# GpSimd takes over sums of weights and products of gated tiles, and the due times around them move

## The reference

```python
out_d = sm_attn(q_d, k_d, v_d)                    # means over 4 positions
attn = softmax(where(|i - j| < 4, scale * q @ k.T, -1e9))
x = (repeat(out_d, 4) + attn @ v)                 # 2304 x 512
x = ((x @ w1) * (x @ w2)) @ w3 @ w_out            # d_ff 1024
h = maximum(maximum(x @ u1, x @ u2), x @ u3)      # d_ff 768
out = h @ u_out
```

## Time and profile before

| | us |
|---|---|
| median of 3 runs | 718.35 (716.84 to 719.42) |
| the profiled execution | 716.85, span 715.1 |
| PE busy | 681.6 (95%) |
| DVE busy | 464.2 (65%) |
| POOL busy | 316.2 (44%) |
| ACT busy | 274.8 (38%) |
| DMA, share of 16 engines | 74.2% |

### The profile page before, as it was taken

The page is one execution under the profiler, slowest core; times in us unless marked ns, Lnnn a source line. Parts: engine busy times, 40 slices in busy tenths (PEclk is TensorE's granted clock), DMA queues, the critical chain, the costliest instruction groups (busy, mean ns, idle before and its releaser), DMA issues.

```text
span 715.1 us, 16905 instructions
## 1 busy us (share of the span) xinstructions
PE 681.6 (95%) x6848; PEld 648.1 (91%) x6848; DVE 464.2 (65%) x843; ACT 274.8 (38%) x590; POOL 316.2 (44%) x280
## 2 busy tenths in 40 slices
PE   8999989799968999989999999999999999999998
PEld 7878878798868999889999999999999999999997
DVE  4465788878877674466545575457775677756673
ACT  5455334434433444356444355123241222412221
POOL 6989354654755422254022235024382243812441
PEclk9999999989999999999999999999999999999999
DMA  9884577778764877997999857996769766697632
GB/s 311 265 276 135 141 211 219 208 211 225 225 170 142 265 229 255 327 313 246 306 349 353 276 205 275 414 399 231 229 231 399 246 220 229 245 406 245 214 142 88
DMA packets 97820, 180.04 MB, mean 252 GB/s; under 512 B 7760, under 2 KB 47952, under 8 KB 96976
## 3 DMA queue, kind: packets, MB, share of 16 engines
q1 hardware_dynamic: 97744, 178.98, 74.2%
HBM read 137.53 MB, written 41.42 MB: 250 GB/s over the span
## 4 chain that ended last, share of the span: by engine, by line
PE 69%; DVE 15%; DMA 6%; issue 3%; ACT 3%; POOL 2%; SPq 2%; DVEq 0%; ACTq 0%
PE psum L825 21%; PE psum L827 20%; PE psum L826 20%; DMA attention<-wb 4%; DVE room L1240 3%; PE psum L835 2%; PE psum L842 2%; PE psum L864 2%; DVE room L1237 1%; ACT attention L1407 1%; DVE room L1238 1%; DMA weights_stream<-attention 1%; POOL weights_split L1631 1%; DVE attention L1097 1%; PE psum L873 1%
## 5 line engine op out<-in xcount | busy, mean ns | idle before, releaser
L1631 POOL TENSOR_TENSOR second_split<-xy,second_split 128x384 fp32r<-128x384 f32 x99 | 104.8, 1077 | 208.9 <-ACT second_split L1407 208.9
L825 PE MATMUL psum<-second_split,weights_split 128*128 128x384 f32 x402 | 135.0, 336 | 0.8 <-DVE sums L1313 0.6
L826 PE MATMUL psum<-second_split,weights_split 128*128 128x384 f32 x402 | 134.3, 334 | 0.0
L827 PE MATMUL psum<-second_split,weights_split 128*128 128x384 f32 x402 | 134.3, 334 | 0.0
L825 PE MATMUL psum<-weights_split 128*128 128x384 f32 x278 | 94.6, 340 | 5.8 <-ACT xy L1407 1.6
L827 PE MATMUL psum<-weights_split 128*128 128x384 f32 x278 | 93.0, 335 | 0.0
L826 PE MATMUL psum<-weights_split 128*128 128x384 f32 x278 | 93.0, 334 | 0.0
L1631 POOL TENSOR_TENSOR weights_split<-xy,weights_split 128x384 fp32r<-128x384 f32 (+1 forms) x65 | 75.2, 1170 | 28.2 <-ACT weights_split L1407 28.1
L825 PEld LDWEIGHTS psum<-second_split,weights_split 128*128 128x128 f32 x402 | 75.5, 188 | 2.7 <-DVE sums L1313 1.5
L826 PEld LDWEIGHTS psum<-second_split,weights_split 128*128 128x128 f32 x402 | 75.5, 188 | 0.0
L827 PEld LDWEIGHTS psum<-second_split,weights_split 128*128 128x128 f32 x402 | 75.5, 188 | 0.0
(11 more groups left out here) (143 smaller groups left out, 1454.2 us busy)
## 6 DMA issues: line engine op xcount, KB each, us to landing
weights_split<-weights_stream SPq DMA_DIRECT2D x39, 768.0 KB, 5.5
weights_split<-gate_weights_stream SPq DMA_DIRECT2D x112, 256.0 KB, 4.6
weights_split<-weights_stream SPq DMA_DIRECT2D x54, 512.0 KB, 6.3
weights_stream<-attention SPq DMA_DIRECT2D x48, 256.0 KB, 3.1
xy<-wa SPq DMA_DIRECT2D x40, 256.0 KB, 5.0
attention<-qk SPq DMA_DIRECT2D x16, 576.0 KB, 4.4
weights_stream<-attention SPq DMA_DIRECT2D x24, 384.0 KB, 2.9
gate_weights_stream<-room SPq DMA_DIRECT2D x16, 448.0 KB, 4.7
```

The lines of the kernel that those rows point to most:

```text
L825: pe.matmul(out, lhs[:, 0], rhs[:, 0], start=first, stop=False, skip_group_check=read_between)
L826: pe.matmul(out, lhs[:, 0], rhs[:, 1], start=False, stop=False, skip_group_check=read_between)
L827: return pe.matmul(out, lhs[:, 1], rhs[:, 0], start=False, stop=last, skip_group_check=read_between)
L1631: return pool.tensor_tensor(out, full, high.bitcast(F32), ALU.subtract)
```

## The change

`combine_wc` moves from DVE to POOL unchanged, due at +0.3 instead of +0.5. The highs of these sums are due at +5 instead of +4, which is 4.7 steps after the sums, the lows at +6 instead of +5.2, the stores at +8.4 instead of +7.8. The multiplications of gated tiles move from `gate_result` to a new `gated_product` on POOL (tiles (0,0), (1,1) and (0,1) for odd q), and the splits behind them are due 0.6 step later on ACT and 0.9 on POOL (0.1 earlier on POOL for tile (1,0)). The last layer starts with the first six f of three groups instead of two. `store_ready` issues its three pieces as three steps 1.05 apart. The due times of `preparations`, `x_activations` and `y_activations` move.

```diff
-    at = [25, 36, 46] + [55.5 + 3.6 * n for n in range(9)] + [91 + 11 * n for n in range(5)] + [145 + 3.3 * n for n in range(7)]
+    at = [25, 36, 46] + [58 + 3.3 * n for n in range(9)] + [91 + 11 * n for n in range(5)] + [147 + 3.3 * n for n in range(7)]
...
-        begin = (max(G_BEGIN - 16, position("x_out", 3 * PAIRS - 1)), G_BEGIN + G_FIRST - 4.8)[s]
+        begin = (max(G_BEGIN - 16, position("x_out", 3 * PAIRS - 1)), G_BEGIN + G_FIRST + 9)[s]
...
-                at += 1.75
+                at += 1.2
...
-    return [(at + (3.5 + i if i < 7 else 11.2 + 0.95 * i) + late, step) for i, step in enumerate(Y_STEPS)]
+    return [(at + (10 + 0.6 * i if i < 7 else 11.4 + 0.8 * i) + late, step) for i, step in enumerate(Y_STEPS)]
...
-                     ("LAST", s, 0, 6, 8), ("LAST", s, 1, 6, 8)) + tuple(("LAST", s, g, 0, 8) for g in range(2, 2 * JO)):
+                     ("LAST", s, 2, 0, 6), ("LAST", s, 0, 6, 8), ("LAST", s, 1, 6, 8), ("LAST", s, 2, 6, 8)) + tuple(
+                         ("LAST", s, g, 0, 8) for g in range(3, 2 * JO)):
...
-                out.append((at + 1.1, ("G", q, tile)))
+                out.append((at + (0.7 if tile == (1, 0) else 1.7), ("G", q, tile)))
...
-                                 [(at, ("GATE_OUT", n)) for n, at in enumerate(gate_preparations(7.8))],
+                                 [(at, ("GATE_OUT", n)) for n, at in enumerate(gate_preparations(8.4))],
...
-                                 [(at, ("READY", n)) for n, at in enumerate(preparations(4))]):
+                                 [(at, ("READY", n, i)) for i in range(len(LOADED)) for n, at in enumerate(preparations(4 + 1.05 * i))]):
...
-                    if n == 0 and g < 2 and f in (0, 6, 7) or f == 0 and g == JO:
+                    if n == 0 and g < 3 and f in (0, 6, 7) or f == 0 and g == JO:
...
-                    dve.wait_ge(g_summed[tile], q + 1)
-                    dve.tensor_tensor(to, to, kept, ALU.mult).then_inc(gated_by[tile], 1)
...
-                                 [(at, ("HIGH_WC", n)) for n, at in enumerate(gate_preparations(4))],
+                                 [(at, ("HIGH_WC", n)) for n, at in enumerate(gate_preparations(5))],
...
+            def combine_wc(n):
+
+                made = gmade_b[n % GMADE]
+                pool.wait_ge(wc_in[n % GMADE], 16 * (n // GMADE + 1))
+                pool.tensor_tensor(made[:, 2, :], made[:, 7, :], made[:, 5, :], ALU.add)
+                pool.tensor_tensor(made[:, 4, :], made[:, 1, :], made[:, 7, :], ALU.subtract).then_inc(gs13_made, 1)
+                pool.wait_ge(gs13_made, n + 1)
+                pool.tensor_tensor(made[:, 0, :], made[:, 2, :], made[:, 1, :], ALU.subtract).then_inc(gs2_made, 1)
+                pool.wait_ge(gs2_made, n + 1)
+                pool.tensor_tensor(made[:, 6, :], made[:, 3, :], made[:, 0, :], ALU.subtract).then_inc(gs_made, 1)
...
+            def gated_product(q, tile):
+                kept = {(0, 0): kept_1, (1, 1): kept_167, (0, 1): kept_16[q % 2]}[tile]
+                pool.wait_ge(g_summed[tile], q + 1)
+                pool.tensor_tensor(results(q, tile), results(q, tile), kept, ALU.mult).then_inc(gated_by[tile], 1)
...
-                                 [(at, ("LOW_WC", n)) for n, at in enumerate(gate_preparations(5.2))],
+                                 [(at, ("COMBINE_WC", n)) for n, at in enumerate(gate_preparations(0.3))],
+                                 [(at, ("LOW_WC", n)) for n, at in enumerate(gate_preparations(6))],
...
-                                 [(at + 0.6, step) for at, step in after_products("G")],
+                                 [(at + 0.5, ("M",) + step[1:]) for at, step in after_products("C") if step[1] % 2 and step[2] != (1, 0)],
+                                 [(at + 0.9, step) for at, step in after_products("G")],
```

More of the change, by code:

```diff
@@ L762, in load_raw, with store_ready @@
                 sp.dma_start(raw_b[n % RAWS], wb[n]).then_inc(wb_in[n % RAWS], 16)
-            def store_ready(n):
+            def store_ready(n, i):
                 u, kp = (n // KP, n % KP) if n < UPS * KP else (UPS + (n - UPS * KP) // FP, (n - UPS * KP) % FP)
                 sp.wait_ge(wb_lo, n + 1)
-                at = 0
-                for es in LOADED:
-                    words = 2 * P * len(es)
-                    sp.dma_start(group_dram(GROUP_OF[(u, es[0])])[:, words * kp:words * (kp + 1)],
-                                 ready_f[n % 2][:, at:at + words]).then_inc(made_out[n % 2], 16)
-                    at += words
+                es = LOADED[i]
+                at, words = 2 * P * sum(len(b) for b in LOADED[:i]), 2 * P * len(es)
+                sp.dma_start(group_dram(GROUP_OF[(u, es[0])])[:, words * kp:words * (kp + 1)],
+                             ready_f[n % 2][:, at:at + words]).then_inc(made_out[n % 2], 16)
             def load_group(i):
@@ L1231, in make_x @@
                 add.then_inc(xs_made, 1)
-            def combine_wc(n):
-                made = gmade_b[n % GMADE]
-                dve.wait_ge(wc_in[n % GMADE], 16 * (n // GMADE + 1))
-                dve.tensor_tensor(made[:, 2, :], made[:, 7, :], made[:, 5, :], ALU.add)
-                dve.tensor_tensor(made[:, 4, :], made[:, 1, :], made[:, 7, :], ALU.subtract).then_inc(gs13_made, 1)
-                dve.wait_ge(gs13_made, n + 1)
-                dve.tensor_tensor(made[:, 0, :], made[:, 2, :], made[:, 1, :], ALU.subtract).then_inc(gs2_made, 1)
-                dve.wait_ge(gs2_made, n + 1)
-                dve.tensor_tensor(made[:, 6, :], made[:, 3, :], made[:, 0, :], ALU.subtract).then_inc(gs_made, 1)
             def gate_result(q, tile):
@@ L1273, in _ @@
                    "H": gate_product, "COMBINE": combine, "LOW_WB": low_wb, "T": lambda i, kp: make_y(0, i, kp),
-                   "C": gate_result, "XT": make_x, "COMBINE_WC": combine_wc}
+                   "C": gate_result, "XT": make_x}
             for step in in_order(unit_jobs(["qk_sum", "down_max", "local_max", "scale_down", "scale_local", "x_out"]),
@@ L1279, in _ @@
                                  after_products("C"),
-                                 [(at, ("COMBINE_WC", n)) for n, at in enumerate(gate_preparations(0.5))],
                                  [(at, ("XT",) + step[1:]) for at, step in x_activations(0.2) if step[0] == "T"],
@@ L1683, in _ @@
             run = {"v_sum": v_sum, "SPLIT": split_w, "SPLIT_X": split_x, "H": h_low,
-                   "E": lambda e, kp: split_y(0, e, kp), "LOW_WC": low_wc, "XE": split_xs,
-                   "G": gated_low}
+                   "E": lambda e, kp: split_y(0, e, kp), "COMBINE_WC": combine_wc, "LOW_WC": low_wc,
+                   "XE": split_xs, "M": gated_product, "G": gated_low}
             of_vector = [("SPLIT", 2 * m + 1) for m in range(EARLY)]
```

## The result

| | before | after |
|---|---|---|
| median, us (9 runs each) | 718.89 (716.84 to 722.75) | 714.98 (711.97 to 718.58) |
| ratio | | 0.9939, 95% interval 0.9911 to 0.9967 |
| profiled execution: span, us | 715.1 | 713.4 |
| VectorE busy, us | 464.2 | 400.2 |
| GpSimd busy, us | 316.2 | 366.8 |

A forecast was written before the change was run, and what follows sets the result against it. It took the units to be slow because VectorE stalls behind GpSimd. Terms -20.8 + 2.0 - 1.7 + 1.3 = -19.2 from 716.85 gave 697.65 us; with the median 1.5 above, forecast 699, range 691 to 709.

The forecast's parts named there:

- Sums of w1 and w2: First MLP beside attention units: moving the sums to GpSimd frees VectorE of 52.6 us and gains PE 20.8 us.
- Round the ring of three: Weight preparations: store landing before the next raw load makes 14.3 us, in three preparations of 7.0; costed at nothing.
- Late `v_sum`: Attention units: with GpSimd fuller, v_sum comes 3 to 4 us late at five or six of ten units; cost 2.0 us.
- Three groups: Start of the last layers: a third group's matmuls remove waits for lows, 2.9 us, and half-speed matmuls, 1.5: gain 4.4.
- Ends: Ends of the last layers: later preparations give back 1.8 us at the second pass; last stage 1.3 later, 0.9 counted.
- Products on GpSimd: Gated tiles: 24 multiplications leave VectorE and cost GpSimd 24 us; nothing either way, or up to 0.3 us at 24 places.
- stores one by one: SyncE's queue: the same 72 issues, one piece at a time; nothing, though ScalarE's high_wb may wait up to 1 us.
- `make_x`: PE's 2.0 us wait behind the make_x adds stays, may grow by 1 or 2; by the lock could reach 4 us.
- B: Rival: GpSimd bounds the units, sums at 0.77 us each, stretch of 135.5 instead of 145; 708 us, chance 0.18.
- C: Rival: preparations at the ends of the passes last 4 us each, PE waits 3 us more at each; 705, chance 0.17.
- D: Rival: slower, since GpSimd's waiting at the head of its queue does not shrink; 726 us, chance 0.06.
- E: Rival: no gain from the sums, for example since waits for x_out come from ScalarE; 716 us, chance 0.04.

The follow-up runs named there:

- e2: Changed kernel with the sums of w1 and w2 back on VectorE: 726.35 us, ratio 1.008 to the kernel before.
- e3: Changed kernel with the raw loads of w1 and w2 due at -3 instead of -4.5: 706.07 us, ratio 0.9811 to the kernel before.
- e5: Kernel before with only the sums (and their highs, lows, stores) moved as in the change, and raw loads due at -3: 703.22 us, ratio 0.9767.
- e9: Kernel before with only the raw loads of w1 and w2 due at -3 instead of -4.5: 718.31 us beside 718.53, ratio 1.001.
- e6: e5 with the last layer begun by three groups: 702.59 us, ratio 0.9754 to the kernel before.
- e7: e3 with the preparations of the second MLP due as before the change: 699.84 us, ratio 0.9717 to the kernel before.
- e8: e7 with the 24 multiplications of gated tiles back on VectorE: 700.24 us, ratio 0.9709 to the kernel before.
- e11: e7 with the raw loads of w1 and w2 due at -2 instead of -3: 697.54 us, ratio 0.9716 to the kernel before.
- e10: e7 with make_x for the first pass begun 3.2 steps later, behind a unit's scaling: 693.32 us, ratio 0.9668 to the kernel before.
- e1: Kernel before with only the sums of w1 and w2 on GpSimd, with the due times that go with them: 711.19 us, ratio 0.9884.

## Why the prediction was wrong, point by point

- **Sums of w1 and w2 (-20.8): the mechanism right, the gain not.** The stalls were real and VectorE lost the time that was forecast. At the ninth unit PE was 11.8 us early, and e2 prices the move at some 10 us in the changed kernel. But by the last unit 4.9 us were left of the 18.8 that stood in the sum. That is 14 of the 17.5 us by which the span missed.
- **The step that failed** is the one on SyncE: "*Round the ring of three: ... = 14.3 us, in three preparations of 7.0. It holds if GpSimd adds under 6 us. Costed at nothing*". The durations in it were near (5.4 us to landing against 4.7, an add of 0.46 against 0.47). The form was not. It counts the ring of three buffers as if the rounds overlapped; but one queue issues all of it in order, and there the store of n - 3 and the load of n that waits for it are mostly neighbours. So the landing is paid in full once per preparation: 0.55 + 0.62 to 1.8 + 0.98 + 4.7 to 5.5 us, 8.4 on average over the 15 intervals, where 7.0 were there. The same text held that `QK` and `V` loads queue behind that wait, which names the victim, and that "*without it each us of wait costs one*". What stands in its place is a wait of 48.2 us in SyncE's queue and 28.5 us of VectorE waiting for q and k. e3 and e5 show it (9 and 8 us for one number), e9 shows why it couldn't be seen before: VectorE's stalls hid it.
- **Late `v_sum` (+2.0): about right.** PE waited 0.6 us for it. GpSimd's load was 113.85 us where 113 were forecast, its add 0.46 where 0.47 were taken. The Trainium skill (GPSIMD Engine Reference, Performance versus the Vector engine) has it some two times slower than VectorE. The rows, which decide here, give 0.46 against 0.29 us undisturbed, 1.6 times; against the mean of 0.82 us that the sums took on VectorE with their stalls, GpSimd is faster.
- **Three groups (-4.4): right as a term** (4.6 in the trace), not seen as a change (e5 to e6, 0.6 us), since both ends of the passes then wait longer for something else.
- **Ends (+1.8 and, with the 0.9 of before, +2.2): the mechanisms right, the sizes small.** The second pass waited for ScalarE's copy behind the last high, as forecast, but 3.28 us: the last high began 3.7 us behind PE's arrival (342.62 against 338.88) where 3.0 were taken (348.5 against 345.5), and the copy was there 1.7 us later where 1.0 was taken. The last stage waited 4.17 us for DMA, where the three groups and the units had brought PE early and 7 preparations 2 steps later had not; 1.5 us of half clock came on top, which the sum did not have. Together 7.9 instead of 4.0. By e7 the later due times were to blame for most of what was lost there.
- **Products on GpSimd, stores one by one: nothing**, as said; for the products e8 agrees, to within a microsecond or two. The stores alone were not tried.
- **`make_x` (2.0 stays, may grow by 1 or 2): right in the changed kernel** (2.03 us). Where SyncE's bound is lifted it is 4.6 in e3, e6, e8 and e11, and 2.0 to 2.1 in e5 and e7. The Trainium skill (SBUF — State Buffer, Who interferes with whom) states an exclusive lock between VectorE's instructions with two SBUF inputs and GpSimd's reads of SBUF. The 6.2 us for four adds in e3, during which GpSimd ran without a pause, agree with it. Moving the adds behind the scaling was worth some 4 us in the end (3.5 to e10 from e7 by the ratios, 4.2 from e11, the clock included).
- **The rivals.** B (GpSimd bounds the units, for a price of 0.77 us a sum) is refuted by the 0.46 us, by e3 and by e10. C (the ends take back more) came true in part, 4 us of its 6. D is out: GpSimd's wait for `h_split` shrank. E (716) is nearest to the time, but by luck: it said that the sums bring nothing, and e1 shows that they bring 8 us. None of the rivals had SyncE, so the range of 691 to 709 left out the time.

## What to carry to other kernels

A removed stall gives only what the next bound leaves, so the queues behind it must be walked in their written order, with every wait charged to all that stands behind it; a ring of buffers whose store and next load are neighbours in one in-order queue cost a full landing each round here. Put other issues between the two, even if that seems to make the load late. And an edit that shows nothing alone (e9) was worth 8 us once the bound in front of it was lifted, so an edit to a hidden bound must be judged again after the one that hides it is gone.

## What the runs showed that was not expected

A raw load due 1.5 steps later was issued up to 9 us earlier (191.8 to 182.8 us for the last of 16).

TensorE's clock did not follow the length of a wait alone. In after, the wait of 3.25 us at 197.5 us was followed by half clock, the one of 3.28 us at 341.1 us was not (stretches of 4 us behind each; the clock is the third number from the end):

```profile
200.00:204.00 4.00, 3.25 (x109) 2.84 (x110) 1.74 (x4) 1.84 (x6) 3.25 (x3) 0.50 0.90 256
...
344.00:348.00 4.00, 3.01 (x16) 2.75 (x17) 2.11 (x6) 1.41 (x4) 0.00 (x0) 1.00 0.97 291
```

0.50 is 1.2 GHz, 1.00 is 2.4. Over the traces of all these kernels the granted clock fell behind every other wait of 3 us or more, behind some of those between 1.7 and 3 us (2.41 at 163 us of after, but not 1.84 at 326 us of e10), and behind none that was shorter; in the 10 us behind such a wait a fall cost 1.4 to 3.1 us of full-speed time, and once, in e2, 4.6. What PE did before the wait at 341 us that it had not done before the others is left open.
